# TensorE's batch program without a loop, and the products of the reciprocals behind the first half of the values

## The chip, the cores and the metric

One core of a Trainium2 chip runs the kernel. The metric is device time in microseconds (us) of one execution. The engines are named as in the profile: PE is TensorE (PEld its weight loads), DVE VectorE, ACT ScalarE, POOL GpSimd, SP SyncE, whose queue issues the transfers.

## What is computed

Attention with rotary position encoding over 4 batches of 8 heads (576 positions, 64 numbers each), then a two-layer feed-forward over the 2304 tokens:

```python
q_rot, k_rot = rotate(q), rotate(k)
scores = 1 / np.sqrt(D) * np.matmul(q_rot, k_rot.transpose(0, 1, 3, 2))
attn = np.exp(scores - np.max(scores, axis=-1, keepdims=True))
attn = attn / (np.sum(attn, axis=-1, keepdims=True) + 1e-09)
x = np.matmul(attn, v)                        # -> (2304, 512)
h = x @ w_in
g = np.maximum(h, 0) + alpha * np.minimum(h, 0)
out = g @ w_out
```

All is float32. Where rounding matters, an operand is split in a high and a low part and the product is taken as three matmuls.

## The kernel before

**Two phases.** The attention goes pair of heads by pair of heads: 4 batches of 4 pairs are 16 periods, p = 0 to 15, and a 17th, p = 16, finishes the last pair and begins the feed-forward. A period computes the scores and exponentials of pair p, the values of pair p - 1, and prepares queries and keys of pair p + 1. The feed-forward follows in 6 chunks of 384 tokens; the change leaves it alone.

**Programs.** Each engine has its own program, written out in order, and the engines meet in semaphores. `batches` (line 294) writes batch 0 out, makes a hardware loop `Fori(1, NB - 1)` of batches 1 and 2, and writes batch 3 out. All engines use it. On PE this is line 812. The loop runs twice, so each engine jumps back once, between p = 7 and p = 8.

**PE's period** (line 701). Nine score tiles of 128 queries are computed: one of the remainders (REM), four of the first head (A0 to A3) and four of the second (B0 to B3). They alternate between two buffers, so a tile's matmuls wait until DVE has read the tile two before it (`max_done`, line 563). Between the tiles stand transposes of the exponentials (`turn_two`, line 671), transposes of queries and keys (`turn`, line 622), the spread of remainders (`spread` of U_MIXED, lines 649 and 652), the values in two halves (`pv`, lines 693 and 697), and the spread of the reciprocal sums over the partitions: `spread` of U_INV, line 644, 16 matmuls. The last is what the text calls the products of the reciprocals.

**Banks.** Results of transposes and spreads go to four PSUM banks. `BANK_OF` gives U_MIXED and U_INV the same bank, 2, and `fill` (line 533) makes PE wait until the unit before in that bank has been copied out. U_MIXED is copied out by ACT (line 843, high part) and then DVE (lines 1016 and 1021, low part and the remainder's reciprocals). DVE does that in its own order: behind the read of score tile A3, and ahead of B0 (lines 1119 to 1130).

**Behind U_INV.** ACT copies the product to `inv_sb` (line 867), behind the exponentials of A3 and ahead of PA0 and of those of B0. DVE multiplies the values by it (`normalise`, line 1066), behind B1.

**The shape of a matmul.** The profile writes 64*128 for one that uses 64 rows of the array and 128 columns, and 128*64 for the other way. Scores of A and B and the transposes are 64*128; values and spreads are 128*64.

Of the kernel before, what the change touches and what calls it, by code (L numbers as in the profile page):

```python
# [23 lines left out]
U_INV = 10  # L24
# [9 lines left out]
def build(nc, q, k, v, w_in, w_out, alpha, cos, sin, eye, out):  # L34
    NB, NH, S, D = q.shape
# [69 lines left out]
    def evac_count(p, u):  # L105

        return tally(p, u, [w for w in range(UNITS) if BANK_OF[w] == BANK_OF[u]])
# [35 lines left out]
    with ExitStack() as ctx:  # L143
# [150 lines left out]
        def batches(eng, batch):  # L294

            batch(0)
            with eng.Fori(1, NB - 1) as b:
                batch(b)
            batch(NB - 1)
# [9 lines left out]
        def is_opening(p):  # L309
            return isinstance(p, int) and p == 0  # L310
# [221 lines left out]
        def _(pe):  # L532
# [19 lines left out]
            def score(p, t, n):  # L552

                if not has_now(p):
                    return
                if is_opening(p) and n > 1:
                    run_in(1)
                s = p * TILES + n
                if n == 0:
                    for u in OF_NEW:  # L560
                        pe.wait_ge(evac[BANK_OF[u]], evac_count(p - 1, u))
                if not (isinstance(s, int) and s < 2):
                    pe.wait_ge(max_done, s - 1)
                tile, par = s_ps[(t * TILES + n) % 2], t % 2
                ahead = isinstance(p, int) and p == 0
                if n == REM_TILE:
                    for j, (qx, kx) in enumerate(SPLIT):
                        for h in range(2):
                            mm = nc.tensor.matmul(tile[:, h, :], q_nat[par][:, qx, QT * P:QT * P + P],  # L569
                                                  k_nat[par][:, kx, REM + h * HALF:REM + (h + 1) * HALF],  # L570
                                                  start=(j == 0), stop=(j == len(SPLIT) - 1))
                    mm.then_inc(scored, 1)
                    return
                if ahead and n in FIRST_TILES:
                    for j, (qx, kx) in enumerate(SPLIT):
                        for h in range(2):
                            mm = nc.tensor.matmul(tile[:, h, :], q_nat[par][LOW, qx, (n - 1) * P:n * P],  # L577
                                                  k_nat[par][LOW, kx, REM + h * HALF:REM + (h + 1) * HALF],
                                                  start=(j == 0), stop=(j == len(SPLIT) - 1))
                    mm.then_inc(scored, 1)  # L580
                    return
                if n == (A_TILES[len(FIRST_TILES)] if ahead else A_TILES[0]):
                    pe.wait_ge(q_swap_in, (p + 1) * SWAPPED)
                    pe.wait_ge(k_swap_in, (p + 1) * SWAPPED)
                head, i = divmod(n - 1, QT)
                of_q = slice(i * P, (i + 1) * P)
                if head == 0:
                    sides = ((LOW, q_nat[par], k_nat[par], slice(REM, REM + HALF)),
                             (HIGH, q_swap[par], k_swap[par], slice(0, HALF)))
                else:  # L590
                    sides = ((LOW, q_swap[par], k_swap[par], slice(0, HALF)),
                             (HIGH, q_nat[par], k_nat[par], slice(HALF, S)))
                for j, (qx, kx) in enumerate(SPLIT):
                    for h, (rows, q_of, k_of, keys) in enumerate(sides):
                        mm = nc.tensor.matmul(tile[:, h, :], q_of[rows, qx, of_q], k_of[rows, kx, keys],  # L595
                                              start=(j == 0), stop=(j == len(SPLIT) - 1))
                mm.then_inc(scored, 1)
# [27 lines left out]
            def spread(p, t, u):  # L625

                if not exists_now(p, u):
                    return
                bank = fill(p, u)
                if u == U_KQREM:  # L630
                    pe.wait_ge(exp_done, (p - 1) * TILES + 1)
                elif u != U_INV and has_next(p):
                    turned_in(p, 1)
                if u != U_KQREM and has_prev(p):
                    pe.wait_ge(inv_done, p)
                pe.sem_inc(pair_filled, 1)
                par = (t - 1) % 2
                if u == U_KQREM:
                    for r in HEADS:
                        mm = nc.tensor.matmul(bank[r, 0:REM], prob_rem[:, QT * P:S], ident[:, r], start=True, stop=True)  # L640
                elif u == U_INV:
                    for i in range(QT):
                        for r, n in zip(HEADS, (A_TILES[i], B_TILES[i])):
                            mm = nc.tensor.matmul(bank[r, i * P:(i + 1) * P], inv[:, par, n:n + 1].to_broadcast([P, D]),  # L644
                                                  ident[:, :], start=True, stop=True)
                else:
                    if has_next(p):
                        for r in HEADS:
                            mm = nc.tensor.matmul(bank[r, 0:P], rot_q[:, QT, r], ident[:, :], start=True, stop=True)  # L649
                    if has_prev(p):  # L650
                        for r in HEADS:
                            mm = nc.tensor.matmul(bank[r, P:P + REM], inv[:, par, 0:1].to_broadcast([P, D]),  # L652
                                                  ident[:, r], start=True, stop=True)
                mm.then_inc(turned, 1)
# [46 lines left out]
            def period(b, t):  # L701

                p = b * PAIRS + t
                spread(p, t, U_KQREM)
                score(p, t, REM_TILE)
                turn(p, t, U_QREM)
                turn(p, t, U_KREM)
                turn_two(p, t, U_PB[0])
                score(p, t, A_TILES[0])
                score(p, t, A_TILES[1])  # L710
                turn_two(p, t, U_PB[2])
                if not is_opening(p):
                    turn(p, t, U_Q)
                if not is_opening(p):
                    turn(p, t, U_K)
                score(p, t, A_TILES[2])
                score(p, t, A_TILES[3])
                if not is_opening(p):
                    spread(p, t, U_MIXED)
                pv(b, t, 0)  # L720
                if not has_now(p):
                    hidden(0, 0, 0)
                score(p, t, B_TILES[0])
                score(p, t, B_TILES[1])
                if is_opening(p):
                    turn(p, t, U_Q)
                    turn(p, t, U_K)
                    spread(p, t, U_MIXED)
                spread(p, t, U_INV)
                turn_two(p, t, U_PA[0])  # L730
                score(p, t, B_TILES[2])
                score(p, t, B_TILES[3])
                turn_two(p, t, U_PA[2])
                pv(b, t, 1)
                if not has_now(p):
                    hidden(0, 0, 1)

            def hidden(i, c, f):

                n = (i * 2 + c) * FT + f  # L740
                if is_first(i, c):
                    if f == 0:
                        pe.wait_ge(exp_done, PERIODS * TILES - 1)
                    pe.wait_ge(w_in_split, 2 * PAIRS + f // (FT // 4) + 1)
                if f == 0:
                    pe.wait_ge(x_split, (i * 2 + c) * 2 * CT + CT)
                if not (isinstance(n, int) and n < 2):
                    pe.wait_ge(neg_done, n - 1)
                cols = slice(f * P, (f + 1) * P)
                step = 0  # L750
                for j in range(CT):
                    for w, xx in ((w_in_hi, x_hi[c % 2]), (w_in_hi, x_lo[c % 2]), (w_in_lo, x_hi[c % 2])):
                        mm = nc.tensor.matmul(h_ps[f % 2], w[:, j, cols], xx[:, j, :],  # L753
                                              start=(step == 0), stop=(step == 3 * CT - 1))
                        step += 1
                mm.then_inc(h_done, 1)
# [51 lines left out]
            def batch(b):  # L808
                for t in range(PAIRS):
                    period(b, t)  # L810

            batches(pe, batch)
            period(NB, 0)
            chunks(pe, chunk)

# [400 lines left out]
```

## Time and profile before

| | us |
|---|---|
| median of three runs | 677.0 |
| lowest and highest of them | 671.92, 677.43 |
| the profiled execution | 672.58 |
| its span, first to last instruction | 670.8 |
| attention, to the start of p = 16 | about 255 |

The profiled execution lies beside the lower of the timed runs. Its granted clock is 0.997 of full speed over the span.

How to read the rows below. A line of the timeline is start, duration, engine, line of the code, operation, output and inputs, count, and in brackets the idle time of that engine before it and what ended it. Merged lines cover several instructions. PE's matmuls are pipelined and their ends are modelled, so distances are best read from start to start of the weight loads (PEld), which come in the program's order with the matmuls. "Issue" is time in which the engine waited for nothing that the profile shows.

### The profile page before, as it was taken

The page shows a single profiled execution, that of the slowest core. Times are in us where ns is not written, and L with a number is a line of the kernel's source. Part 1 is how long each engine was busy: PE and PEld are TensorE (multiplying, and loading weights), DVE is VectorE, ACT ScalarE, POOL GpSimd, SP SyncE. Part 2 cuts the span into 40 slices and gives each one's busy share as a digit, 9 for nine tenths or more (in the row PEclk, how much of TensorE's full clock was granted, in tenths as well). Part 3 has the DMA queues.
Part 4 walks back from the last instruction along what each step waited for, and adds up shares of the span by engine and source line. Part 5 has one row for each costly group of instructions (what it writes and reads, how often), then busy time and mean ns, then how long its engine had stood idle before and what let it go on. Part 6 is the DMA issues. An engine that isn't in the chain of part 4 may idle for free.

```text
span 670.8 us, 15166 instructions
## 1 busy us (share of the span) xinstructions
PE 656.0 (98%) x5570; PEld 561.7 (84%) x5570; DVE 338.8 (51%) x779; ACT 320.7 (48%) x730; POOL 266.8 (40%) x254
## 2 busy tenths in 40 slices
PE   8899999999999998999999999999999999999998
PEld 7677787777877776898899999999999999999996
DVE  4687777767888764445522332233233323332222
ACT  2788888868888875333332223222322232223223
POOL 3766788858865323222222222222222222222222
PEclk9999999989999999999999999999999999999999
DMA  6596554444554336000010001000100010001001
GB/s 148 153 229 178 124 136 110 106 105 103 120 121 104 83 117 251 1 1 1 1 48 0 1 1 47 1 1 0 47 0 0 0 47 0 0 0 48 1 0 48
DMA packets 73311, 41.62 MB, mean 62 GB/s; under 512 B 59812, under 2 KB 64292, under 8 KB 72740
## 3 DMA queue, kind: packets, MB, share of 16 engines
q1 hardware_dynamic: 72978, 40.62, 23.1%
q8 instruction: 42, 0.69, 0.4%
q10 hardware_dynamic: 274, 0.16, 0.1%
q14 instruction: 17, 0.14, 0.1%
HBM read 22.95 MB, written 4.72 MB: 41 GB/s over the span
## 4 chain that ended last, share of the span: by engine, by line
PE 94%; ACT 2%; DVE 1%; issue 1%; DMA 0%; SPq 0%; POOL 0%; ACTq 0%; DVEq 0%
PE banks L753 30%; PE banks L782 30%; PE banks L697 9%; PE banks L595 8%; PE banks L671 5%; PE banks L622 3%; PE banks L693 3%; PE banks L644 2%; PE banks L569 2%; PE banks L649 1%; ACT prob L824 1%; ACT pt L867 1%; DMA cos_sb<-in_cos 0%; PE banks L577 0%; PE banks L652 0%
## 5 line engine op out<-in xcount | busy, mean ns | idle before, releaser
L517 POOL TENSOR_TENSOR g_lo<-g,g_hi 128x384 fp32r<-128x384 f32 (+1 forms) x98 | 99.7, 1018 | 309.2 <-ACT g_hi L936 299.8
L1100 DVE TENSOR_SCALAR g<-banks,alpha_sb 128x384 f32<-128x384 f32 (+1 forms) x98 | 59.7, 610 | 250.9 <-ACT pos L927 250.9
L753 PE MATMUL banks<-x_hi,w_in_lo 128*128 128x384 f32 x384 | 129.3, 337 | 0.0
L753 PE MATMUL banks<-x_hi,w_in_hi 128*128 128x384 f32 x384 | 129.2, 337 | 0.0
L753 PE MATMUL banks<-x_lo,w_in_hi 128*128 128x384 f32 x384 | 129.0, 336 | 0.0
L927 ACT ACTIVATE pos<-banks 128x384 f32<-128x384 f32 x96 | 47.1, 491 | 170.2 <-PE banks L753 170.2
L782 PE MATMUL banks<-w_out_hi,g_hi 128*128 128x512 f32 x288 | 114.9, 399 | 0.3
L782 PE MATMUL banks<-w_out_hi,g_lo 128*128 128x512 f32 x288 | 112.9, 392 | 0.0
L782 PE MATMUL banks<-w_out_lo,g_hi 128*128 128x512 f32 x288 | 111.9, 388 | 0.0
L936 ACT ACTIVATE g_hi<-g 128x384 fp32r<-128x384 f32 (+1 forms) x98 | 50.9, 519 | 115.9 <-DVE g L1103 115.9
L824 ACT ACTIVATE prob<-prob,nmax 128x576 f32<-128x576 f32 x128 | 98.2, 773 | 1.3 <-DVE prob L991 1.2
L991 DVE TENSOR_SCALAR_CACHE_REDUCE prob<-banks 128x576 f32<-128x576 f32 x128 | 92.8, 752 | 11.1 <-PE banks L595 9.6
L753 PEld LDWEIGHTS banks<-x_hi,w_in_hi 128*128 128x128 f32 x384 | 72.1, 188 | 4.5 <-issue 0.9
L753 PEld LDWEIGHTS banks<-x_lo,w_in_hi 128*128 128x128 f32 x384 | 72.2, 188 | 3.5
L867 ACT ACTIVATE pt<-banks 128x512 f32<-128x512 f32 x112 | 61.6, 596 | 24.3 <-PE banks L622 21.9
L753 PEld LDWEIGHTS banks<-x_hi,w_in_lo 128*128 128x128 f32 x384 | 72.2, 188 | 0.0
L697 PE MATMUL banks<-pt,raw_v 128*64 128x288 f32 x512 | 67.6, 406 | 0.0
L595 PE MATMUL banks<-k_nat,q_nat 64*128 64x288 f32 x375 | 67.3, 310 | 0.1
L595 PE MATMUL banks<-k_swap,q_swap 64*128 64x288 f32 x375 | 66.9, 310 | 0.0
L782 PEld LDWEIGHTS banks<-w_out_hi,g_lo 128*128 128x128 f32 x288 | 54.1, 188 | 13.8
L782 PEld LDWEIGHTS banks<-w_out_hi,g_hi 128*128 128x128 f32 x288 | 54.1, 188 | 9.7 <-issue 1.4
L782 PEld LDWEIGHTS banks<-w_out_lo,g_hi 128*128 128x128 f32 x288 | 54.1, 188 | 8.3
(80 smaller groups left out, 917.3 us busy)
## 6 DMA issues: line engine op xcount, KB each, us to landing
q_swap<-q_nat SPq DMA_DIRECT2D x32, 256.0 KB, 3.7
k_swap<-k_nat SPq DMA_DIRECT2D x32, 144.0 KB, 3.1
out<-stage SPq DMA_DIRECT2D x18, 256.0 KB, 2.0
raw_q<-in_q SPq DMA_DIRECT2D x32, 128.0 KB, 2.9
raw_k<-in_k SPq DMA_DIRECT2D x32, 128.0 KB, 2.5
raw_v<-in_v SPq DMA_DIRECT2D x32, 128.0 KB, 2.3
w_in_raw<-in_moe_w_in SPq DMA_DIRECT2D x4, 1024.0 KB, 5.8
w_out_raw<-in_moe_w_out SPq DMA_DIRECT2D x8, 512.0 KB, 7.5
```

The lines of the kernel that those rows point to most:

```text
L517: nc.gpsimd.tensor_tensor(g_lo[f % 2][:, part], g[f % 2][:, part], g_hi[f % 2][:, part].bitcast(F32), ALU.subtract).then_inc(g_lo_done, 1)
L595: mm = nc.tensor.matmul(tile[:, h, :], q_of[rows, qx, of_q], k_of[rows, kx, keys], start=(j == 0), stop=(j == len(SPLIT) - 1))
L671: mm = nc.tensor.transpose(bank[:, to:to + D], prob[r, i, first + w * P:first + (w + 1) * P], ident[r, r])
L697: mm = nc.tensor.matmul(o[own, :], raw_v[par][:, j, own], pt[:, pt_slot(par, head, j), cols], start=False, stop=(j == QT - 1))
L753: mm = nc.tensor.matmul(h_ps[f % 2], w[:, j, cols], xx[:, j, :], start=(step == 0), stop=(step == 3 * CT - 1))
L782: mm = nc.tensor.matmul(y_ps[c % 2][m], lhs[j][f % 2][:, m * P:(m + 1) * P], rhs[j][:, f, :], start=(f == 0 and j == 0), stop=(f == FT - 1 ...
L824: nc.scalar.activation(row_of(n), row_of(n), ACT.Exp, scale=-1.0, bias=nmax[:, t % 2, n:n + 1], accum_out=rsum[:, t % 2, n:n + 1]).then_in ...
L867: ins = nc.scalar.activation(dst, src, ACT.Copy)
L927: nc.scalar.activation(pos[f % 2][:, :], h_ps[f % 2], ACT.Relu).then_inc(pos_done, 1)
L936: nc.scalar.activation(g_hi[f % 2][:, part], g[f % 2][:, part], ACT.Copy).then_inc(g_hi_done, 1)
L991: nc.vector.tensor_scalar(row_of(n), s_ps[(t * TILES + n) % 2], -SCALE, None, ALU.mult, ALU.min, accum_out=nmax[:, t % 2, n:n + 1]).then_i ...
L1100: nc.vector.tensor_scalar(g[f % 2][:, part], h_ps[f % 2][:, part], 0.0, alpha_sb[:, f:f + 1], ALU.min, ALU.mult).then_inc(neg_done, 1)
```

## The change

PE's four batches are written out one behind the other instead of partly in a loop; the other engines keep their loop. And the products of the reciprocals move in PE's period, from behind B1 to directly behind the first half of the values, ahead of B0. In p = 0 they don't exist, and in p = 16, where there are no B tiles, their order against the rest stays as it was.

```diff
@@ -720,13 +720,13 @@
                 pv(b, t, 0)
                 if not has_now(p):
                     hidden(0, 0, 0)
+                spread(p, t, U_INV)
                 score(p, t, B_TILES[0])
                 score(p, t, B_TILES[1])
                 if is_opening(p):
                     turn(p, t, U_Q)
                     turn(p, t, U_K)
                     spread(p, t, U_MIXED)
-                spread(p, t, U_INV)
                 turn_two(p, t, U_PA[0])
                 score(p, t, B_TILES[2])
                 score(p, t, B_TILES[3])
@@ -809,7 +809,8 @@
                 for t in range(PAIRS):
                     period(b, t)
 
-            batches(pe, batch)
+            for b in range(NB):
+                batch(b)
             period(NB, 0)
             chunks(pe, chunk)
```

## Rows read from the trace of the kernel before

**Rows 1.** Page of the profile: busy time, and the chain that ended last.
```profile
PE 656.0 (98%) x5570; PEld 561.7 (84%) x5570; DVE 338.8 (51%) x779; ACT 320.7 (48%) x730; POOL 266.8 (40%) x254
...
PE 94%; ACT 2%; DVE 1%; issue 1%; DMA 0%; SPq 0%; POOL 0%; ACTq 0%; DVEq 0%
```

**Rows 2.** Timeline of the weight loads: starts of p = 4, 8, 12 and 16.
```profile
72.89 0.39 PEld L640 LDWEIGHTS banks<-ident,prob_rem 128*64 128x64 f32 x4
...
130.67 1.84 PEld L697 LDWEIGHTS banks<-pt,raw_v 128*64 128x64 f32 x16
135.25 0.23 PEld L640 LDWEIGHTS banks<-ident,prob_rem 128*64 128x64 f32 x4 [2.73 <-issue]
...
151.35 0.39 PEld L640 LDWEIGHTS banks<-ident,prob_rem 128*64 128x64 f32 x4
...
195.95 0.39 PEld L640 LDWEIGHTS banks<-ident,prob_rem 128*64 128x64 f32 x4
...
254.90 0.39 PEld L640 LDWEIGHTS banks<-ident,prob_rem 128*64 128x64 f32 x4
```

**Rows 3.** Busy time by stretch: each engine, then PE's granted clock, DMA share, GB/s.
```profile
136.00:138.00 2.00, 2.00 (x24) 1.72 (x25) 0.27 (x1) 0.00 (x0) 0.36 (x1) 0.57 0.24 50
...
256.00:258.00 2.00, 1.21 (x32) 1.12 (x33) 1.04 (x4) 1.17 (x3) 1.34 (x2) 1.00 0.93 272
```

**Rows 4.** Timeline of ACT and DVE across the jump back, and ACT at p = 12.
```profile
138.16 1.57 ACT L867 ACTIVATE pt<-banks 128x512 f32<-128x512 f32 x3 [4.58 <-PE banks L622]
...
135.65 0.23 DVE L1041 COPY pt<-banks 128x64 f32<-128x64 f32 x1 [1.30 <-PE banks L640]
...
198.15 1.57 ACT L867 ACTIVATE pt<-banks 128x512 f32<-128x512 f32 x3 [1.23 <-PE banks L622]
```

**Rows 5.** Timeline of the weight loads in p = 12, behind the first half's values.
```profile
202.06 1.84 PEld L697 LDWEIGHTS banks<-pt,raw_v 128*64 128x64 f32 x16
204.34 0.18 PEld L595 LDWEIGHTS banks<-k_swap,q_swap 64*128 64x128 f32 x1 [0.44 <-DVE prob L991]
205.32 0.85 PEld L644 LDWEIGHTS banks<-ident,inv 128*64 128x64 f32 x16 [0.17 <-issue]
206.35 0.58 PEld L671 LDWEIGHTS banks<-ident,prob 64*128 64x128 f32 x16 [0.17 <-issue]
```

**Rows 6.** The same in p = 11, from the products to PA2.
```profile
191.57 0.57 PEld L671 LDWEIGHTS banks<-ident,prob 64*128 64x128 f32 x16 [0.17 <-issue]
192.06 0.19 PEld L595 LDWEIGHTS banks<-k_swap,q_swap 64*128 64x128 f32 x1
...
193.03 0.61 PEld L671 LDWEIGHTS banks<-ident,prob 64*128 64x128 f32 x16
```

**Rows 7.** Timeline of DVE in p = 12: reads of the scores, low parts, B0.
```profile
197.99 0.76 DVE L991 TENSOR_SCALAR_CACHE_REDUCE prob_rem<-banks 128x576 f32<-128x576 f32 x1 [0.18 <-PE banks L622]
...
204.52 0.21 DVE L1021 COPY inv_sb<-banks 128x64 f32<-128x64 f32 x1
205.03 0.76 DVE L991 TENSOR_SCALAR_CACHE_REDUCE prob<-banks 128x576 f32<-128x576 f32 x1 [0.30 <-PE banks L595]
205.72 0.08 DVE L991 DVE_READ_ACCUMULATOR prob<-banks 128x1 f32 x1
```

**Rows 8.** The copy of line 1021 and the first weight load of B0 in p = 15.
```profile
246.95 0.22 DVE L1021 COPY inv_sb<-banks 128x64 f32<-128x64 f32 x1
...
248.54 0.18 PEld L595 LDWEIGHTS banks<-k_swap,q_swap 64*128 64x128 f32 x1 [0.44 <-issue]
```

**Rows 9.** PE released by DVE: the copy that ends, and the weight load behind.
```profile
13.28 0.29 DVE L1016 TENSOR_TENSOR k_nat<-banks,k_nat 128x128 fp32r<-128x128 f32 x1
13.69 0.82 PEld L569 LDWEIGHTS banks<-k_nat,q_nat 128*128 128x128 f32 x6 [0.46 <-issue]
...
255.36 0.46 DVE L1066 TENSOR_TENSOR x<-banks,inv_sb 128x288 f32<-128x288 f32 x1 [1.54 <-PE banks L697]
256.04 0.35 PEld L622 LDWEIGHTS banks<-ident,prob_rem 64*128 64x128 f32 x8 [0.76 <-issue]
```

## The prediction

> **What bounds the kernel.** I read the busy times and the chain first: PE is busy 98% of the span and is 94% of the chain that ended last, so only what shortens or interrupts PE's order counts [rows 1]. Then the timeline of PE's weight loads, period by period. Two things are to be seen there. The jump back between p = 7 and p = 8 shows as a hole [rows 2]. And within a period PE has almost no hole, but DVE runs close behind it: in p = 12 DVE waits for PE at the read of REM (197.99) and then works without a pause until the copy of line 1021 ends at 204.52 + 0.21 = 204.73 [rows 7], while PE's first weight load of B0 stands at 204.34 [rows 5]. Both parts of the change act at these places.
>
> **Part one: no loop on PE.** The weight loads of the values end at 130.67 + 1.84 = 132.51. In other periods the next load follows 0.10 later, so 132.61 was due and 135.25 came: 2.64 us [rows 2]. Behind the hole the granted clock is 0.57 from 136 to 138, near the lower of its two levels, 1.2 of 2.4 GHz [rows 3]; period 8 takes 151.35 - 135.25 = 16.10 us. The four periods from 12 to 15, written out, take 254.90 - 195.95 = 58.95, or 14.74 each [rows 2]. Period 8 thus lost a further 1.36, most of it to the clock. Together that is 4.0 us. An upper bound comes from the whole loop: 195.95 - 72.89 = 123.06 for eight periods against 8 x 14.74 = 117.92, that is 5.1; the 1.1 above the 4.0 is spread over the other seven and may belong to the other engines' loops, which stay. I take 4.3.
>
> The lower bound of the gain asks what is late next. DVE, which also jumps here, was through and waited 1.30 us for PE [rows 4], so its jump is no cover. ACT's jump lies in an idle time of 4.58 [rows 4]; in p = 12, with no jump, it idles 1.23 there, so a jump of ACT longer than that would take some of the gain. Since DVE's left room for 1.30 us of waiting, I take ACT's to be as short. The lower bound is 0.
>
> The Trainium skill (Runtime: NRT & Kernel Launch, Instruction fetch mechanics) says that instructions are fetched ahead in order only, and that a jump out of the pages held stalls until its target is fetched. By that, written-out code has no such hole; the trace agrees in p = 1 to 3 and 12 to 15, which are written out and show none, and in the one of 2.64 at the jump.
>
> **Part two: what the move takes away.** In p = 12 the order of weight loads is: values end 203.90, B0 204.34, products 205.32, PA0 206.35 [rows 5]. There are three holes before these, 0.44, 0.17 and 0.17. They stand where the shape changes between 128*64 and 64*128, and none such stands between two groups of one shape (at most 0.10). Behind the move the shape changes once, from products to B0, instead of three times. Kept: 0.17. Gone: 0.34 + 0.17 and a little more, about 0.5 us a period if nothing else waited.
>
> **What it adds, first wait.** The products go to the bank of U_MIXED, and PE must wait until line 1021 has copied it out. DVE's copy ends at 204.73, and two cases show 0.12 (13.57 to 13.69) and 0.22 (255.82 to 256.04) from DVE's end to PE's load [rows 9]. I take 0.10, as the first, and 0.22 as the bound. The products then begin at about 204.83 instead of a free 204.00. DVE can't come sooner: its chain starts at a result of PE and the values' end is not in it. Behind the waiting PE are all B tiles.
>
> **What it adds, second wait.** The products lay between B1 and B2 and gave DVE time. Now only PA0 is between. From the products' first load to the next group is 206.35 - 205.32 = 1.03 [rows 5], so B0 loads at 205.85. DVE's read of B0 begins 0.69 behind its first load (204.34 to 205.03) and ends 0.77 later (205.72 + 0.08) [rows 5, 7]: 205.85 + 0.69 + 0.77 = 207.31. B2 needs it and loads at 207.41. By PE alone it would be 205.85 + 0.97 + 0.49 = 207.31, with the 0.97 of two tiles and the 0.49 of PA0 [rows 6]. B3 needs the read of B1, which ends 0.68 behind that of B0, at 207.99; it loads at 208.09, where PE alone would have been ready at about 207.89. PA2 follows 0.47 later, half of 0.97 and what a change would add left out: 208.56. Before, PA2 would come at 206.35 + 0.49 + 0.97 = 207.81 by the same rows [rows 5, 6]. So the period grows by 0.75 us.
>
> With 0.22 for both waits in place of 0.10 it grows by about 1.0. With the first wait wholly absent, products at 204.00, all later times are 0.83 earlier, and the growth is -0.08: even then the read of B1 holds B3, and almost nothing of the 0.5 is left. These are the bounds: -0.1 to 1.0 a period.
>
> Nothing behind PA2 gives it back. DVE scales the first values behind B1's read, done near 208.4, and the second half of the values loads near 209.2; ACT's chain from PA0 on moves by about 0.5 us, less than PE's, so its last exponential comes early enough. Its earlier product and the earlier scaling by DVE gain nothing, as PE waits for neither.
>
> **How many.** In 14 periods, 1 to 14, the low parts are there. In eleven of them the copy ends 0.36 to 0.43 behind B0's first load, as in p = 12; in three of the loop, 5, 7 and 11, it is 0.07 to 0.25. In p = 15 no pair is prepared, and the copy ends at 247.17 [rows 8], over a microsecond before B0's first load at 248.54 [rows 8]: no first wait, growth 0. In p = 16 the order stays. 14 x 0.75 = 10.5 us, with bounds of -1 and 14. The three shorter distances may lie at 0.4 once PE is written out; if they stay, take off 0.6.
>
> **The sum.** +10.5 - 0.3 (half of that 0.6) - 4.3 = +5.9 us. Against the profiled execution, 672.6, this is 678.5 us; against the median of the runs, 677.0, it is 682.9. The profiled one sits with the lowest of the three runs, the other two are 5 us above; I can't tell where the next runs fall, and put the forecast between, at 681.
>
> **The rivals.**
>
> *The waits cost more.* With 0.22 per release, 14 us less 4.3 is +10, or 685. For it: p = 16 showed 0.22. Against it: a plain release showed 0.12. Chance 0.17.
>
> *The gain of the loop is taken by another engine's jump.* ACT's idle time of 4.58 could hide one of over 1.2 us [rows 4]. Then PE's hole stays in part, up to all 4.3: +6 to +10, near 684. Against it: DVE's was short. Chance 0.12.
>
> *The move costs nothing, the loop's gain stays.* This is the case on the other side. The place is bank 2: if the copy of line 1021 were through when the values end, 203.90, the first wait would go and the period would be as long as before. It decides from a DVE 0.9 us earlier. Result -4 to -5, or 670. Against it: eleven periods with the same 0.4, and DVE without a pause. Chance 0.12.
>
> *The holes of shape go, and stay gone.* If the first wait were absent and B3's wait as well, each of 15 periods gains 0.5: -7.5 - 4.3 = -12, or 667 (between both bases). Two things of DVE speak against it, so 0.08. The Trainium skill (TensorEngine Tiling (Array Packing), Key Properties) has the rule behind this rival: changing the tiling mode drains the engine. The trace agrees, with holes of 0.44 and 0.17 at the changes.
>
> *The clock falls in each period.* Holes of 0.6 plus 0.1 plus 0.2 us could bring the lower clock, and a period would lose about the 1.36 of p = 8: +19 more. Against it: between 256 and 258 PE is busy only 1.21 of 2 us and the clock stays at 1.00 [rows 3]. Chance 0.03.
>
> **How the numbers follow.** The forecast has 0.48. Faster or slower by over 1% is over 6.8 us, about what a measurement of this kernel can tell from no change. My sum of +5.9 lies just inside, so of the 0.48 I put 0.30 inside and 0.18 above. Within 1%: 0.30 + 0.12 (move for nothing) + 0.04 (a part of the other engine's jump) = 0.46. Slower: 0.18 + 0.17 + 0.08 + 0.03 = 0.46. Faster: 0.08. The likeliest case's own range is 675 to 686, which is +3 to +8 on either base. The range for 8 in 10 goes from 671, which takes in most of the move for nothing, to 688, which holds the dearer waits on the median's base; it leaves out the gained holes, the clock, and the edge of the others.
>
> **What would show it.** The products (line 644) stand behind line 697, with a hole of 0.8 to 1.0 us in the weight loads released by line 1021, in 14 periods and not in the last two. B0 to B3 show PE waiting for line 991, 0.1 to 0.3 us a period, where before nothing waited. Periods 1 to 14 are near 15.5 us, p = 15 stays near 14.7. The hole at p = 8 and the stretch at the lower clock are gone. The feed-forward is as long as before. I am wrong in the first wait if line 644 follows the values within 0.2 us; wrong in the second if B3's load follows B2's by 0.5 in all periods; wrong in part one if a hole of over 1 us stands at the start of p = 8, and its releaser tells whose jump it is. If the growth is right and the time is not, the runs' own level differs from that of the profile.

## The result

The changed kernel takes 679.6 us (median of 13 runs, 678.25 to 681.47) against 674.1 us before (median of 13, 671.92 to 677.43). The ratio is 1.0079, with an interval of 1.0057 to 1.01: slower by 5.3 us. Its profiled execution spans 676.4 us, 5.6 us more than the 670.8 of before. The forecast was +5.9 us, or 681 us.

The page's chain that ended last shows where to look: PE has gone from 94% to 81%, and DVE from 1% to 12% [rows 1]. Lines behind 812 count one more in the changed kernel, so line 1021 is 1022 there and 991 is 992.

```profile
PE 656.4 (97%) x5570; PEld 561.3 (83%) x5570; DVE 331.6 (49%) x779; ACT 320.9 (47%) x730; POOL 266.6 (39%) x254
...
PE 81%; DVE 12%; issue 4%; ACT 1%; DMA 0%; SPq 0%; DVEq 0%; POOL 0%
```

PE works as long as before (656.4 against 656.0). What is new is waiting. The view of who waited for whom, on PE's matmuls, has a line that the kernel before doesn't have: 14 waits of at most 0.6 us at the products. On the weight loads the same 14, with the one of p = 16, are 14.2 us, for there the distance counts from the last load and not from the end of a long matmul. A line of this view gives the total of the waits, their number and the longest.

```profile
PE banks L644 <- DVE inv_sb L1022: 7.3, 14, 0.6
...
PEld banks L644 <- issue: 14.2, 15, 1.0
PEld banks L622 <- issue: 7.0, 19, 2.6
PEld banks L595 <- DVE prob L992: 4.2, 17, 0.3
```

The timeline of the weight loads, with the starts of p = 4, 8, 12, 15 and 16 (compare [rows 2]), and for p = 12 the loads from the first half of the values to PA2 (compare [rows 5, 6]):

```profile
75.57 0.39 PEld L640 LDWEIGHTS banks<-ident,prob_rem 128*64 128x64 f32 x4
...
137.49 0.39 PEld L640 LDWEIGHTS banks<-ident,prob_rem 128*64 128x64 f32 x4
...
199.55 0.39 PEld L640 LDWEIGHTS banks<-ident,prob_rem 128*64 128x64 f32 x4
...
205.65 1.84 PEld L697 LDWEIGHTS banks<-pt,raw_v 128*64 128x64 f32 x16
208.45 0.88 PEld L644 LDWEIGHTS banks<-ident,inv 128*64 128x64 f32 x16 [0.96 <-issue]
209.50 0.18 PEld L595 LDWEIGHTS banks<-k_swap,q_swap 64*128 64x128 f32 x1 [0.17 <-issue]
210.28 0.65 PEld L671 LDWEIGHTS banks<-ident,prob 64*128 64x128 f32 x16
...
211.71 0.18 PEld L595 LDWEIGHTS banks<-k_swap,q_swap 64*128 64x128 f32 x1 [0.25 <-DVE prob L992]
212.08 0.66 PEld L671 LDWEIGHTS banks<-ident,prob 64*128 64x128 f32 x16
...
246.04 0.39 PEld L640 LDWEIGHTS banks<-ident,prob_rem 128*64 128x64 f32 x4
260.72 0.39 PEld L640 LDWEIGHTS banks<-ident,prob_rem 128*64 128x64 f32 x4
```

The products (line 644) now stand directly behind the values (line 697), 0.96 later, and ahead of B0 (line 595 at 209.50). B3 loads at 211.71, PA2 at 212.08. From p = 4 to p = 8 are 137.49 - 75.57 = 61.92 us, or 15.48 a period, and the hole at p = 8 is gone. Period 15 takes 14.68. Over the eight periods that were PE's loop, 4 to 11, the changed kernel needs 123.98 us and the old one 123.06: here the loop's gain and the waits' cost nearly cancel.

DVE in the same period (compare [rows 7]). Its copy ends at 208.12 + 0.21 = 208.33, and PE's products load 0.12 later. Its read of B1 ends at 211.57 + 0.08 = 211.65, and PE's B3 loads 0.06 later:

```profile
208.12 0.21 DVE L1022 COPY inv_sb<-banks 128x64 f32<-128x64 f32 x1
210.21 0.76 DVE L992 TENSOR_SCALAR_CACHE_REDUCE prob<-banks 128x576 f32<-128x576 f32 x1 [1.88 <-PE banks L595]
210.90 0.08 DVE L992 DVE_READ_ACCUMULATOR prob<-banks 128x1 f32 x1
210.90 0.75 DVE L992 TENSOR_SCALAR_CACHE_REDUCE prob<-banks 128x576 f32<-128x576 f32 x1
211.57 0.08 DVE L992 DVE_READ_ACCUMULATOR prob<-banks 128x1 f32 x1
```

### The profile page after: what moved, and what is told of

Its sections match the earlier page's. It is cut to its first block, busy times and chain, and to the rows that moved or that the text cites. A ratio compares the mean times of both kernels' runs of the same rounds, so it can differ in the third digit from the quotient of the medians.

```text
span 676.4 us, 14995 instructions
## 1 busy us (share of the span) xinstructions
PE 656.4 (97%) x5570; PEld 561.3 (83%) x5570; DVE 331.6 (49%) x779; ACT 320.9 (47%) x730; POOL 266.6 (39%) x254
## 4 chain that ended last, share of the span: by engine, by line
PE 81%; DVE 12%; issue 4%; ACT 1%; DMA 0%; SPq 0%; DVEq 0%; POOL 0%
PE banks L753 30%; PE banks L782 29%; PE banks L595 6%; PE banks L697 5%; DVE prob L992 4%; PE banks L644 3%; PE banks L671 2%; PE banks L569 2%; DVE pt L1042 2%; DVE k_nat L1017 2%; PE banks L693 2%; DVE prob_rem L992 2%; DVE q_nat L1017 1%; PE banks L622 1%; PE banks L550 1%
## 5 line engine op out<-in xcount | busy, mean ns | idle before, releaser
L595 PE MATMUL banks<-k_nat,q_nat 64*128 64x288 f32 x375 | 71.2, 314 | 0.1
L595 PE MATMUL banks<-k_swap,q_swap 64*128 64x288 f32 x375 | 70.7, 313 | 0.2
```

## Experiments

Times are compared with runs of the kernel before on the same chip. Where it says one execution, there is one time and one profile, and what is read from it is the distance between the starts of periods, which in undisturbed periods repeats within 0.1 us. The first period is left out of what is said on periods, since in some profiles the lower clock of the opening reaches into it.

### The two parts apart

**Only written out.** PE's batches are written out, the products stay at their old place.

```diff
-            batches(pe, batch)
+            for b in range(NB):
+                batch(b)
```

> PE's batches written out, the products at their old place. Theory: the hole of 2.64 us at the start of p = 8 and the slow stretch behind it go, all periods from 4 to 15 take 14.7 to 14.8 us, and the kernel is 4 to 5 us faster than before (ratio 0.993). Rival (another engine's own jump is late next): a hole of over 1 us stays at the start of p = 8, released by ACT or DVE, and less than 2 us are gained.

Measured: 669.5 us, ratio 0.9913 (0.9887 to 0.9938), which is 5.9 us faster (4.2 to 7.6). The timeline of the weight loads has no hole at p = 8, and the periods 4 to 11 take 191.32 - 73.25 = 118.07 us, 5.0 less than before:

```profile
73.25 0.39 PEld L640 LDWEIGHTS banks<-ident,prob_rem 128*64 128x64 f32 x4
...
132.39 0.39 PEld L640 LDWEIGHTS banks<-ident,prob_rem 128*64 128x64 f32 x4
...
191.32 0.39 PEld L640 LDWEIGHTS banks<-ident,prob_rem 128*64 128x64 f32 x4
```

So no other engine's jump was late next, and the gain is the full 5.0, not the 4.3 that I took. This kernel and the two below that differ from it only in a loop (669.5 and 669.3 us) are the fastest complete ones of the study; they can't be told apart.

**Only moved.** The products stand at their new place, PE's loop is kept.

```diff
                 pv(b, t, 0)
                 if not has_now(p):
                     hidden(0, 0, 0)
+                spread(p, t, U_INV)
                 score(p, t, B_TILES[0])
...
-                spread(p, t, U_INV)
                 turn_two(p, t, U_PA[0])
```

> The products moved, PE's loop kept. Theory: 14 periods grow by 0.75 us, the hole at p = 8 stays at about 2.6 us with its slow clock, and the kernel is 10 to 11 us slower than before (ratio 1.016). Rival (the two parts share a cost, for instance since DVE gains on PE during the hole): clearly less than 10 us, with a shorter wait in p = 8 and 9.

Measured: 683.8 us, ratio 1.0118 (1.0092 to 1.0143), 8.0 us slower (6.2 to 9.7). That is less than the 10 to 11 expected. The two parts do not add. The growth of 0.75 is there in the periods outside the loop, 4.5 us in six of them, but the eight periods of the loop take only 3.0 more than before (126.09 against 123.06): in this order the loop costs less. A second execution of the same kernel was to tell why.

> Only the products moved, PE's loop kept, once more for its profile. In the first profile the loop cost 2.1 us in this order, all of it the hole, against 5.0 in the old order. Theory (in the new order PE has idle time in each period, so what the loop adds within a period is hidden, and the clock behind the hole is a matter of phase): the hole is 2.0 to 3.0 us again, periods 4 to 7 and 9 to 11 take 15.48 to 15.51, and period 8 takes 15.5 or, with the slow clock, up to 17. Rival (the new order itself keeps the clock up): 1.00 behind the hole again.

Starts of p = 4, 8, 9 and 12 in that execution:

```profile
76.28 0.39 PEld L640 LDWEIGHTS banks<-ident,prob_rem 128*64 128x64 f32 x4
...
140.22 0.23 PEld L640 LDWEIGHTS banks<-ident,prob_rem 128*64 128x64 f32 x4 [2.07 <-issue]
156.88 0.39 PEld L640 LDWEIGHTS banks<-ident,prob_rem 128*64 128x64 f32 x4
...
203.34 0.39 PEld L640 LDWEIGHTS banks<-ident,prob_rem 128*64 128x64 f32 x4
```

The six other periods of the loop take 15.48 to 15.49, no more than in the changed kernel. In the old order the loop's periods other than 8, without the hole, took 14.8 to 15.1 against 14.74, about 1 us in all; in the new order nothing of it is left, so the new waits cover it. The hole is 2.1 here and 2.2 in the first profile, against 2.7 in the rows of before. And period 8 took 16.66 here, 1.2 too long with a clock of 0.50 behind the hole, and 15.55 in the first profile, where the clock stayed at 1.00. The clock is thus a matter of the execution. Why the hole itself is 0.5 to 0.9 us smaller than in the two profiles of the kernel before (2.73 and, below, 2.94) isn't shown.

Both executions have another hole, which was not expected. In p = 15, where the prediction has no growth, the period takes 15.56 us against 14.65 before and 14.68 in the changed kernel. The weight loads of the products stop for 0.87 us behind the twelfth of sixteen, in the first execution:

```profile
257.63 0.85 PEld L644 LDWEIGHTS banks<-ident,inv 128*64 128x64 f32 x12
259.35 0.24 PEld L644 LDWEIGHTS banks<-ident,inv 128*64 128x64 f32 x4 [0.87 <-issue]
```

The second has it at the same load, again with 0.87. PE's code is written out there, and the kernel has no wait inside these sixteen matmuls. The other ten profiles, the changed kernel's among them, have no such hole, so this belongs to the program with the moved products and the loop together. Its cause is open.

**The kernel before once more.**

> The kernel before once more, for its profile. The hole at p = 8 is 2.0 to 2.8 us again. Open is the clock behind it: if it falls to about 0.57 for some 4 us again, period 8 takes 16.1; if it stays at 1.00, as in the run with only the products moved, period 8 takes 14.8 to 15.0, and the 1.4 us of it belong to the phase of the clock gate in the one profile.

Measured in one execution: a hole of 2.94 in the weight loads, a little above the expected range, and a period 8 of 16.04 with the same slow clock behind it. Here the lower clock came both times. The 1.36 us of the prediction repeat as 1.3, and periods 4 to 6 and 9 to 11 at 14.81 to 14.96 too.

### Is the hole the jump?

**A loop that runs once.** Batch 1 alone is in the loop, 2 and 3 are written out.

```diff
-            batches(pe, batch)
+            batch(0)
+            with pe.Fori(1, 2) as b:
+                batch(b)
+            batch(2)
+            batch(3)
```

> The kernel before, but PE's loop holds batch 1 alone and runs once; batches 2 and 3 are written out. So the program still has a loop and waits on registers, but doesn't jump back. Theory (the hole is the jump back, after which the target's instructions are fetched): no hole at p = 8, periods 8 to 15 of 14.73 to 14.8 us, and periods 4 to 7 together at most 1 us over 4 x 14.74, by which it is seen what the register waits cost. Rival (leaving a loop, or the batch boundary of the other engines, makes the hole): a hole of 2 us or more at p = 8.

Measured in one execution: 669.5 us, no hole at p = 8, periods 4 to 7, those of the loop, in 132.44 - 73.40 = 59.04 us (4 x 14.74 is 58.96), and all periods behind at 14.61 to 14.77. The period starts agree with those of the written-out kernel within 0.2 us. Without a jump back there is no hole. The profile counts 14998 instructions against 14995 written out and 15166 with the loop of two passes, so the builder may have made constants of the loop's one value. This run is then nearly the written-out program, and shows neither what waits on registers cost by themselves nor what entering and leaving a loop cost. For the last the kernel before has an answer: it enters its loop at p = 4 (72.89) and leaves it at p = 12 (195.95), both without a hole in the weight loads [rows 2]. Only the jump back has one.

**The feed-forward's loop written out too.**

```diff
-            chunks(pe, chunk)
+            for i, c in ((0, 0), (0, 1), (0, 2), (1, 1), (1, 2), (2, 1)):
+                chunk(i, c)
```

> PE's batches written out with the products at their old place, and PE's feed-forward chunks written out as well, so that PE's program has no loop at all. Theory (a jump costs only where PE has no queue of long matmuls to live on; the feed-forward's jump shows no hole over 0.5 us in the trace of before): within 0.5 us of the run with the batches written out alone, the feed-forward's stretch as long as before. Rival (every jump costs some 2.6 us): 2 to 3 us faster than that run.

Measured: 669.3 us, ratio 0.9924 (0.9895 to 0.9953), with the batches alone 0.9913: the same within the intervals. From the start of p = 16 to the end are 668.1 - 252.41 = 415.7 us, and 670.8 - 254.90 = 415.9 before. A jump there costs nothing that can be measured: in the kernel before, which has it, the weight loads show no hole of 0.2 us or more from 330 to 662 us. Why the attention's jump costs and this one doesn't is not shown. PE had not just waited there: the sixteen value loads before the hole follow each other about every 0.11 us (16 loads in 1.84 us from 130.67 on [rows 2]). Two things differ that no run separates. In the feed-forward a load comes every 0.17 to 0.23 us, and its loop body is shorter, 672 matmuls against 854 recorded in four attention periods.

### Which wait costs

**Another bank.** The products go to bank 0. U_Q and U_K share banks 0 and 1, so PE waits for the copies of both; DVE does these ahead of A3. PA0 to PA3 take the banks in another order, to keep free what is needed.

```diff
-BANK_OF = (1, 2, 3, 0, 1, 2, 3, 0, 1, 2, 2, 0, 1, 2, 0)
+BANK_OF = (1, 2, 3, 0, 1, 2, 3, 0, 1, 2, 0, 2, 1, 0, 2)
@@ spread
                 bank = fill(p, u)
+                if u == U_INV:
+                    pe.wait_ge(evac[BANK_OF[U_K]], evac_count(p, U_K))
```

> As the changed kernel, but the products go to bank 0, which the low parts of queries and keys have left by then (PE waits for these), and the transposes of the first head go round the banks in another order. Theory: the hole of 1 us before the products goes, the wait of B3 for DVE's read of B1 stays near 0.25 us, and a period takes 14.65 to 14.75 as with the products at their old place: the time is that of the run with PE written out alone, within 1 us. Rival A (the two saved changes of shape are kept): periods of 14.25 us and 7 us less than that. Rival B (the products wait for the reciprocals or for something else than the bank): periods stay at 15.5 us, the time that of the changed kernel.

Measured: 671.6 us, ratio 0.9938 (0.9918 to 0.9958). Periods 2 to 14 take 14.72 to 14.83. The median is 2.1 us above that of the kernel only written out (669.5), where 1 was expected. The profiles don't show this: from the start of p = 1 to that of p = 16 are 221.95 us here and 222.05 there, and the profiled execution took 669.97. What made the other executions longer is open. The timeline of the weight loads in p = 12 (line 646 is the products, 699 the values, 673 the transposes):

```profile
199.33 1.84 PEld L699 LDWEIGHTS banks<-pt,raw_v 128*64 128x64 f32 x16
201.27 1.04 PEld L646 LDWEIGHTS banks<-ident,inv 128*64 128x64 f32 x16
202.48 0.18 PEld L595 LDWEIGHTS banks<-k_swap,q_swap 64*128 64x128 f32 x1 [0.17 <-issue]
203.25 0.64 PEld L673 LDWEIGHTS banks<-ident,prob 64*128 64x128 f32 x16
...
204.68 0.18 PEld L595 LDWEIGHTS banks<-k_swap,q_swap 64*128 64x128 f32 x1 [0.25 <-DVE prob L994]
205.06 0.65 PEld L673 LDWEIGHTS banks<-ident,prob 64*128 64x128 f32 x16
```

The products follow the values within 0.10, and the whole 0.75 us a period is gone. The wait of B3 is still there. So, with the control below, the bank is the cause of the loss, and the move without it is worth nothing, as the lower bound of the prediction had it (-0.08): periods as long as with the products at their old place. The holes of shape did not come back as a gain. Of the 0.5 us, about 0.2 goes into the products themselves, whose loads take 1.04 behind the values and 0.85 at their old place, and B3's wait takes the rest, as the run with short reads will show.

**The control for the banks.** The same banks, products at their old place.

> PE written out, the banks as in the run before, the products at their old place behind B1. A control for the banks alone. All theories: the time of the run with PE written out alone, within 1 us, periods of 14.7 us. If it is slower by more, the new order of the banks has a cost of its own that the run with the moved products carries too.

Measured: 670.2 us, ratio 0.9928 (0.9901 to 0.9954), periods 2 to 14 of 14.70 to 14.80. The order of the banks has no cost of its own.

**The low parts first.** The changed kernel, with DVE's order turned round at one place.

```diff
-                maxima(p, t, A_TILES[3])
                 if not is_opening(p):
                     lo(p, U_MIXED, t)
+                maxima(p, t, A_TILES[3])
```

> The changed kernel, but DVE takes the low parts of U_MIXED and the copy of line 1021 ahead of the read of score tile A3. Nothing else changes. Theory (the first wait is DVE's turn at bank 2): that copy ends 0.5 to 0.7 us earlier, the hole before the products shrinks from about 1.0 to 0.3 to 0.5 us, a period takes 14.85 to 15.05 us instead of 15.49, and the kernel is 6 to 9 us faster than the changed one, near the kernel before. Rival (PE waits for something else at that place, the reciprocals or ACT): periods stay at 15.5 us. Rival (A3's later read stops B1): periods of over 15.2 us.

Measured: 671.7 us, ratio 0.998 (0.9958 to 1.0002) to the kernel before, which puts it some 6.7 us below the changed one (ratio 1.0079); 6 to 9 were expected. Periods 2 to 14 take 14.96 to 15.00 us, but for one of 15.26, p = 9. The copy ends at 201.18 + 0.21 = 201.39 in p = 12, and the products load 0.12 later. The hole is 0.44 in place of 0.96:

```profile
201.51 0.88 PEld L644 LDWEIGHTS banks<-ident,inv 128*64 128x64 f32 x16 [0.44 <-issue]
202.56 0.18 PEld L595 LDWEIGHTS banks<-k_swap,q_swap 64*128 64x128 f32 x1 [0.17 <-issue]
...
201.18 0.21 DVE L1022 COPY inv_sb<-banks 128x64 f32<-128x64 f32 x1
```

With the same bank and the same place, only by DVE's turn, the hole shrinks by 0.52 and the period by 0.52. That is the mechanism from its other side. A3's later read stops nothing.

**Short reads.** The run with the other bank, with less for DVE to read in B0 and B1. It leaves out the scaling and the maximum of half of each of these tiles.

```diff
+                some = slice(0, 1) if n in B_TILES[:2] and not is_opening(p) else slice(0, 2)
-                nc.vector.tensor_scalar(row_of(n), s_ps[(t * TILES + n) % 2], -SCALE, None, ALU.mult, ALU.min,
+                nc.vector.tensor_scalar(row_of(n)[:, some, :], s_ps[(t * TILES + n) % 2][:, some, :], -SCALE, None,
+                                        ALU.mult, ALU.min,
```

> The kernel with the products in bank 0 at their new place, but DVE reads only half of the score tiles B0 and B1 (periods 1 to 15), so the other half isn't scaled and not in the maximum: this part of the computation is left out, to make DVE's reads shorter. Theory (B3 waits for DVE's read of B1, and that holds back what the fewer changes of shape would give): the wait of 0.25 us before B3 goes, and a period takes 14.45 to 14.65 us instead of 14.75. Rival (B3's wait is no cost): still 14.75. Rival (the full 0.5 us of the holes is free then): 14.25.

Measured in one execution: outside the loop of the other engines, periods 2, 3 and 12 to 14 take 14.43 to 14.47, and 14.78 to 14.83 with full reads, 0.35 more. So B3's wait did hold back 0.35 us, and the 14.25 of the full 0.5 is not reached. In periods 5 to 11 it stays at 14.73 to 14.82, and another wait has come up: PE's transposes of the exponentials (line 673) stand 0.29 behind the last loads, in p = 8:

```profile
134.33 0.33 PEld L622 LDWEIGHTS banks<-ident,prob 64*128 64x128 f32 x8
134.95 0.60 PEld L673 LDWEIGHTS banks<-ident,prob 64*128 64x128 f32 x16 [0.29 <-issue]
```

It is DVE that holds PE there. The transposes write banks 0 and 1, and bank 1 is free when DVE has copied out the remainders' spread (line 1046). In p = 8 that copy ends at 134.67 + 0.21 = 134.88 and the loads come 0.07 later; so it is in p = 5 and 7 to 11, within 0.08. Ahead of this copy DVE adds a small number to the row sums (line 1056, 128x9). That addition takes 0.97 to 1.05 us in these periods, and 0.17 in p = 2 to 4 and 14, where the copy is through 0.5 to 0.6 us before the loads. In the slow ones POOL also splits the feed-forward's first weights; that this makes the addition slow isn't shown.

## Why the prediction was right

**Part one, the jump.** Sum: 2.64 for the hole, 1.36 for the period behind it, 4.3 taken with a share of what the loop's other periods lose. Measured: 5.0 in the traces, 5.9 (4.2 to 7.6) in the runs. The mechanism held. The 1.36 was in part luck: it is mostly the lower clock behind the hole, which came in both profiles of this kernel, but not in one of two of the kernel with the products moved. The size was 0.7 low: I gave most of the 1.0 us spread over the loop's other periods to the other engines' loops, and it belonged to PE's, since it went when only PE's was written out. The Trainium skill (Runtime: NRT & Kernel Launch, Instruction fetch mechanics) has instructions fetched ahead in order only, so that a jump to one that isn't held stalls. The traces agree for the attention's jump, with 2.1 to 2.9 us, while the feed-forward's shows no stall that costs time; the fetch itself is seen in no profile. And that written-out code has no hole is not true throughout, by the 0.87 us in p = 15 of the kernel with only the products moved. The rival of another engine's jump fell.

**Part two, what the move takes away.** I counted the holes of shape as 0.5 us that would be gone if nothing waited. The places were right, the worth was not: with the wait gone, the products' own loads behind the values took 0.19 longer. A hole behind a change of shape may partly be the end of the long value matmuls, which whoever stands behind them pays for; the 0.19 fits that, but doesn't prove it. With DVE's reads shortened, 0.35 of the 0.5 did come. The time of the rival that keeps all of it has an error of its own: 12 us below the middle of the two bases is 663, not 667.

**The first wait.** Predicted: products 0.93 behind the last load of the values, by 0.10 from DVE's end to PE's load. Measured: 208.45 - 207.49 = 0.96, with 0.12. It is shown to be bank 2 and DVE's turn at it by two experiments.

**The second wait.** Counted from the end of the values' loads, the prediction had B0, B3 and PA2 at 1.95, 4.19 and 4.66; measured in p = 12 are 2.01, 4.22 and 4.59. B2 was to wait for the read of B0. It came 0.05 behind the end of that read, but also 0.10 behind PA0's loads, the distance without a wait, so that it waited can't be read. Growth of a period: 0.75 predicted, 15.49 - 14.74 = 0.75 measured; periods 2 to 14 lie at 15.47 to 15.57. Period 15 grew by 0.0, as said, and the feed-forward didn't change. In the three periods with distances of 0.07 to 0.25, 5, 7 and 11, the hole before the products is as large as in the others (1.02 to 1.03), so the 0.3 taken off for them was not due.

**The sum.** From the start of p = 1 to that of p = 16 the kernel before takes 226.8 us, the one only written out 222.05 and the changed one 232.0. That is -4.8 for the loop and +9.9 for the moved products, +5.1 together, and the runs say +5.3 (3.8 to 6.7). The forecast had -4.3 and +10.2. The 9.9 is below 14 x 0.75 because the kernel only written out has two long periods of its own, p = 2 with 15.22 and p = 6 with 14.90; against the one with the feed-forward written out too, which lacks the first of them, periods 2 to 14 grew by 9.8, or 0.75 each. A difference of 1% was said to be about what a measurement can tell; thirteen runs of each kernel told 0.8% from nothing. The clock did not fall in the new holes, as the row of 256 to 258 let one expect [rows 3].

**The level of the runs.** The forecast stood between two bases, at 681 - 5.9 = 675.1, and all runs of before have their median at 674.1. The middle was taken because nothing told where the next runs would fall; that it came out within 1.0 us is luck. The traces show where such a spread can come from. The start of p = 1 lies between 27.8 and 30.5 us in the profiles of this study, and the two profiles of the kernel before have it at 28.1 and 30.4, though nothing ahead of it was changed.

## What to carry to other kernels

A matmul group that is moved takes its bank's history along: ask which copy must be through before it may write, and where in its engine's order that copy stands. A group between two double-buffered tiles is cover for their reader, and the price of taking it away is read from start of load to start of read to end of read, here 0.7 + 0.8 us per tile. Two parts of a change should be costed in the order in which they will run together: over its eight periods the loop cost 5.0 us in the old order, and 2.1 and 3.1 us in the order in which PE waits in every period.

## What the runs showed of the hardware

A jump back in PE's program of four attention periods left a hole of 2.1 to 2.9 us in the weight loads in four profiles. One in the feed-forward, where PE's matmuls take 336 to 399 ns each, left none of 0.2 us or more.

The granted clock fell in some executions and not in others with the same waits. Behind the hole of p = 8 it fell in three of four profiles that have it. In the kernel with only the batches written out it fell in p = 16, with PE busy 1.28 and 1.18 of 2 us before, and stayed at 1.00 in p = 16 of the kernel before, at about the same busy times (1.35, 1.00 and 1.30 of 2 us from 255 to 261). Busy time of each engine by stretch, with PE's clock, as in [rows 3]:

```profile
252.00:254.00 2.00, 1.28 (x36) 1.08 (x32) 0.69 (x1) 1.58 (x3) 1.71 (x2) 1.00 0.91 331
254.00:256.00 2.00, 1.18 (x12) 0.86 (x12) 1.49 (x4) 1.92 (x5) 0.00 (x0) 0.94 1.03 386
256.00:258.00 2.00, 2.00 (x10) 1.17 (x8) 1.29 (x3) 0.85 (x2) 0.00 (x0) 0.50 1.04 399
258.00:260.00 2.00, 2.00 (x11) 1.12 (x8) 0.00 (x0) 0.00 (x0) 0.00 (x0) 0.71 0.97 361
```

It cost that profile 1.5 us from p = 16 to the end (417.4 against 415.9). The profiles of the one-pass loop and the first one of the kernel with only the products moved have the same fall (417.4 and 417.3); the other nine have none and take 415.7 to 415.9. With the 2.7 us by which the start of p = 1 differs, this is nearly as large as the effect that was to be measured, and a comparison by period starts was far sharper than one by spans.
